# Decay attention and two MoE layers on one core: one scan chain per pair of chunks, three joins, one normalised block per chunk

## The reference, cut to what matters

```python
batch, n_heads, seq, head_dim = (4, 8, 768, 48)
mag = np.sqrt(a_re * a_re + a_im * a_im)
scale = np.minimum(mag, 0.999) / (mag + 1e-06)
a_re_n, a_im_n = (a_re * scale, a_im * scale)
for t in range(S):
    ar, ai = (a_re_n[:, :, t, :, None], a_im_n[:, :, t, :, None])
    new_re = ar * S_re - ai * S_im
    new_im = ar * S_im + ai * S_re
    S_re, S_im = (new_re + kv, new_im)      # kv: outer product of k[t] and v[t]
    y[:, :, t] = einsum('bhd,bhde->bhe', q[:, :, t], S_re)
x = y, tokens by features (3072 x 384)
h = np.maximum(np.maximum(x @ w1, x @ w2), x @ w3);  x = h @ w_out
# then a second MoE: each token to the one of 8 experts that its logits pick, times a gate
```

## Time and profile before

| | |
|---|---|
| Median of three runs | 1024.53 us |
| The profiled execution | 1025.89 us |
| Its span in the trace | 1024.0 us |
| TensorE matmul busy | 858.9 us (84% of the span) |
| VectorE busy | 649.9 us (63%) |
| GpSimd busy | 481.0 us (47%) |
| ScalarE busy | 450.2 us (44%) |
| From `y_copy(23)` to the end | 656.3 to 1024.0 us |

### The profile page before, as it was taken

The page is one execution under the profiler, slowest core; times in us unless marked ns, Lnnn a source line. Parts: engine busy times, 40 slices in busy tenths (PEclk is TensorE's granted clock), DMA queues, the critical chain, the costliest instruction groups (busy, mean ns, idle before and its releaser), DMA issues.

```text
span 1024.0 us, 18210 instructions
## 1 busy us (share of the span) xinstructions
PE 858.9 (84%) x6326; PEld 770.8 (75%) x6327; DVE 649.9 (63%) x1050; ACT 450.2 (44%) x834; POOL 481.0 (47%) x868
## 2 busy tenths in 40 slices
PE   1236576779898989979998999956999999999995
PEld 1235475678787878868897889856888888888885
DVE  5998866897797888849556665237522352546722
ACT  5751563555555545533444333222422342445621
POOL 1168988996089939963992000004221222323321
PEclk9556887889998999989999999985999999999998
DMA  9104144415233241403211111142711132415410
GB/s 297 57 19 120 51 100 112 113 65 150 77 91 92 74 98 52 102 32 85 62 37 44 37 37 38 63 176 74 278 43 34 46 121 79 157 43 171 152 38 31
DMA packets 42245, 90.78 MB, mean 89 GB/s; under 512 B 6312, under 2 KB 23728, under 8 KB 40768
## 3 DMA queue, kind: packets, MB, share of 16 engines
q1 hardware_dynamic: 38080, 77.48, 24.9%
q0 software_dynamic: 4096, 12.40, 3.8%
HBM read 70.20 MB, written 18.48 MB: 87 GB/s over the span
## 4 chain that ended last, share of the span: by engine, by line
PE 45%; POOL 23%; DVE 16%; issue 5%; DMA 5%; ACT 4%; SPq 1%; ACTq 0%; DVEq 0%; POOLq 0%
POOL c_re L1817 7%; POOL c_im L1818 6%; POOL ring L1820 5%; POOL ring L1821 5%; PE mm L1511 5%; PE yu L1511 4%; PE tr L1511 4%; PE mm L1515 4%; PE tr L1515 4%; PE tr L1512 4%; PE mm L1512 4%; PE yu L1512 4%; PE yu L1515 4%; PE mm L1736 3%; DMA ring<-an_scratch 2%
## 5 line engine op out<-in xcount | busy, mean ns | idle before, releaser
L1511 PE MATMUL mm<-up_hi,x_hi 128*128 128x384 f32 x432 | 162.0, 375 | 64.6 <-DVE h_sb L1064 45.7
L1512 PE MATMUL mm<-up_lo,x_hi 128*128 128x384 f32 x432 | 150.8, 349 | 0.0
L1511 PEld LDWEIGHTS mm<-up_hi,x_hi 128*128 128x128 f32 x432 | 84.8, 196 | 81.8 <-DVE h_sb L1064 51.5
L1817 POOL TENSOR_TENSOR c_re<-ring 112x128 f32<-112x128 f32 (+1 forms) x160 | 106.3, 665 | 67.8 <-DMA ring<-an_scratch 43.8
L1904 POOL DMA_INDIRECT out_rows<-g_o,rows_out x30 | 34.7, 1158 | 184.0 <-DVE g_o L1445 184.0
L900 ACT ACTIVATE g_h<-tr 128x512 f32<-128x512 f32 x60 | 35.9, 598 | 171.2 <-PE tr L1515 149.1
L1064 DVE TENSOR_TENSOR h_sb<-mm,h_sb 128x384 f32<-128x384 f32 x96 | 53.1, 553 | 85.3 <-PE mm L1515 83.1
L1818 POOL TENSOR_TENSOR c_im<-ring 112x128 f32<-112x128 f32 (+1 forms) x160 | 103.4, 647 | 0.0
L1515 PE MATMUL mm<-up_hi,x_lo 128*128 128x384 f32 x432 | 103.2, 349 | 0.0
L1820 POOL TENSOR_TENSOR ring<-c_re,c_im 112x64 f32<-112x64 f32 (+1 forms) x160 | 84.1, 526 | 12.5
L1512 PEld LDWEIGHTS mm<-up_lo,x_hi 128*128 128x128 f32 x432 | 85.4, 198 | 0.0
(11 more groups left out here) (223 smaller groups left out, 1998.4 us busy)
## 6 DMA issues: line engine op xcount, KB each, us to landing
raw<-in_moe_w SPq DMA_DIRECT2D x16, 1536.0 KB, 9.0
a_dn<-in_a_laid SPq DMA_DIRECT2D x20, 384.0 KB, 7.4
an_scratch<-a_dn SPq DMA_DIRECT2D x20, 384.0 KB, 2.3
ring<-an_scratch SPq DMA_DIRECT2D x20, 384.0 KB, 5.6
q_in<-in_q_laid SPq DMA_DIRECT2D x24, 224.0 KB, 3.0
k_in<-in_k_laid SPq DMA_DIRECT2D x24, 224.0 KB, 3.2
v_in<-in_v_laid SPq DMA_DIRECT2D x24, 192.0 KB, 3.3
x_scratch<-x_sb SPq DMA_DIRECT2D x24, 192.0 KB, 2.4
```

The costliest lines, as they stand in the source:

```text
L1511: nc.tensor.matmul(out, hi[:, x, :], w_hi(x), start=(x == 0), stop=False)
L1512: nc.tensor.matmul(out, hi[:, x, :], w_lo(x), start=False, stop=False)
L1817: nc.gpsimd.tensor_tensor(c_re[:, 0:count, :, :], cur, bc(prev[:, :, 0, :], 2, 2), ALU.mult).then_inc(chain_prod, 1)
```

## The change

- Every group from 2 on has its own chain of 15 steps; the double chain of two groups is gone. 157 chain steps instead of 160.
- Every group from 2 on has three joins: six more joins on VectorE (24 instructions).
- The joins of a group stand in three places. Groups 5 and up: the first behind `k_decay` in chunk 2g-3, the second behind the mask of chunk 2g-2, the third behind `k_decay` in chunk 2g-2. Groups 2 to 4: the first behind the mask of chunk 2g-2, the two others behind `k_decay` of that chunk.
- From chunk 4 on, and in chunk 2, one block is normalised in a chunk (before: two in chunks 0 to 4, then one). Block m of chunk n is n+7; the last, 23, falls in chunk 16 instead of 14.
- Ring loads of groups 4 and 6 to 11 stand one or two chunks later in SyncE's program, in chunk 2g-5.
- GpSimd: `turns(g-1)` stands behind step 12 of chain g.
- VectorE: the first late join stands ahead of `norm_inverse`; `moe_max(n-1, 1, 1)` stands ahead of the second late join and of the rotation.
- Start: blocks 2 and 3 are summed ahead of the joins of group 0 and applied (scaled) ahead of `z_newton(0)`, `q_decay(0)` and `k_decay(0)`; `up_low(0)` moves into chunk 0.

```diff
-            if g < SINGLE:
-                return ring_b[:, g % RING, :, :, :, :]
-            return ring_q[:, g // 2 % 2, :, :, :, :]
+            return ring_b[:, g % RING, :, :, :, :]
...
         def norms_in(n):
-            if n < 5:
-                return (2 * n + 4, 2 * n + 5)
-            return (n + 9,) if n + 9 < NORMS else ()
-
-        joins_early = {1: 1}
-        joins_late = {2: 2, 4: 3, 6: 4, 8: 5, 10: 6, 11: 7, 14: 8, 15: 9, 18: 10, 19: 11}
+            first = 2 * n + 4 if n < 2 else n + 6 if n < 4 else n + 7
+            count = 2 if n in (0, 1, 3) else 1
+            return tuple(m for m in range(first, first + count) if m < NORMS)
+
+        joins_early = {1: [(1, b) for b in range(7)]}
+        joins_late = {}
+        for g in range(DIRECT, NG):
+            joins_early[2 * g - 2] = [(g, 0 if g < 5 else 1)]
+            joins_late[2 * g - 2] = [(g, 1), (g, 2)] if g < 5 else [(g, 2)]
+            if g >= 5:
+                joins_late[2 * g - 3] = [(g, 0)]
...
-        ring_at = {max(g - 1, 2 * g - 7): g for g in range(DIRECT, NG)}
+        ring_at = {(g - 1 if g < 4 else 4 if g == 4 else 2 * g - 5): g for g in range(DIRECT, NG)}
...
+            norm_rsqrt(2, norm_of(2))
+            norm_rsqrt(3, norm_of(3))
             split_dn()
             act.wait_ge(s_const, 1)
             stage_z(0)
             z_square(0)
-            norm_rsqrt(2, norm_of(2))
-            z_recip(0)
-            norm_rsqrt(3, norm_of(3))
             norm_rest(2, norm_of(2))
             norm_rest(3, norm_of(3))
+            z_recip(0)
...
+                for g, number in late[:1]:
+                    join(g, number)
                 for m in norms:
                     norm_inverse(m, norm_of(m))
-                if late is not None:
-                    for number in range(apart, len(joins_of(late))):
-                        join(late, number)
+                if prev:
+                    moe_max(n - 1, 1, 1)
+                for g, number in late[1:]:
+                    join(g, number)
                 if more:
                     rotation(n + 1)
-                if prev:
-                    moe_max(n - 1, 1, 1)
...
-            for g in range(SINGLE, NG, 2):
-                if g > SINGLE:
-                    turns(g - 2)
-                chain_steps(g, range(1, 17))
-                turns(g - 1)
-                chain_steps(g, range(17, HALF // 2))
-            turns(NG - 2)
+            for g in range(DIRECT + 1, NG):
+                chain_steps(g, range(1, 13))
+                turns(g - 1)
+                chain_steps(g, range(13, BLK))
             turns(NG - 1)
```

More of the change, by code:

```diff
@@ L449, in chain_of @@
                 return ring_8[:, g, :, :, :, :]
-            if g < SINGLE:
-                return ring_b[:, g % RING, :, :, :, :]
-            return ring_q[:, g // 2 % 2, :, :, :, :]
+            return ring_b[:, g % RING, :, :, :, :]
         def steps_of(g):
             return list(chain_of(g).shape)[2] - 1
-        chains = [g for g in range(1, NG) if g < SINGLE or g % 2 == 0]
         def steps_before(g):
-            return sum(steps_of(c) for c in chains if c < g)
+            return sum(steps_of(c) for c in range(1, g))
         def joins_of(g):
@@ L467, in joins_of @@
                 return [(ring_8[:, g, b, :, :, :], ring_8[:, g, b - 1, 7, :, :]) for b in range(1, 8)]
-            if g < SINGLE:
-                return [(ring_b[:, g % RING, b, :, :, :], ring_b[:, g % RING, b - 1, BLK - 1, :, :]) for b in range(1, NBLK)]
-            return [(ring_b[:, g % RING, b, :, :, :], ring_b[:, g % RING, 1, BLK - 1, :, :]) for b in (2, 3)]
+            return [(ring_b[:, g % RING, b, :, :, :], ring_b[:, g % RING, b - 1, BLK - 1, :, :]) for b in range(1, NBLK)]
         def joins_before(g):
@@ L1181, in _ @@
                 ending = norms_in(n - 1) if 1 <= n <= NC else ()
-                late = joins_late.get(n)
-                apart = 0 if n in (2, 10) else 1
+                late = joins_late.get(n, ())
                 if prev2:
@@ L1202, in _ @@
                     norm_m2(m, norm_of(m))
-                if n in joins_early:
-                    for number in range(len(joins_of(joins_early[n]))):
-                        join(joins_early[n], number)
+                for g, number in joins_early.get(n, ()):
+                    join(g, number)
                 if n == 0:
+                    up_low(0)
                     up_low(1)
@@ L1211, in _ @@
                     up_low(2)
-                if late is not None:
-                    for number in range(apart):
-                        join(late, number)
                 if prev:
@@ L1811, in chain_steps @@
                         pool.wait_ge(pads_loaded, 16 * min(RING, max(RING - DIRECT, g - 1)))
-                        for x in range(g, g + (1 if g < SINGLE else 2)):
-                            pool.wait_ge(ring_loaded[x % RING], 32 * (x // RING + (1 if x % RING >= DIRECT else 0)))
+                        pool.wait_ge(ring_loaded[g % RING], 32 * (g // RING + (1 if g % RING >= DIRECT else 0)))
                     count = list(of.shape)[1]
```

27 lines of the change are left out of this document (8 added, 19 removed).

## The result

| | before | after |
|---|---|---|
| time, median of 4 runs (us) | 1024.4 (1023.4 to 1025.8) | 998.4 (997.2 to 999.0) |
| profiled execution: time, span (us) | 1025.9, 1024.0 | 998.1, 996.4 |
| mean granted clock of TensorE | 0.917 | 0.958 |

The ratio is 0.974 (95% interval 0.973 to 0.976): 2.6% faster, 26.0 us. The forecast was 1002, 3.6 us too high.

The account below looks back on a forecast made before the run. TensorE's floor of 21.6 us a chunk bounds the kernel, with losses above it from waits for VectorE and chains. Terms 0 - 0.6 + 12.1 + 12.0 = 23.5 us off 1025.9 gave 1002.4, forecast 1002, range 989 to 1018.

Parts of the forecast that it names:

- The start: Stretches 0 and 1: first scores about 4.5 us later, chain 1 about 5 earlier; 0 for `y_copy(1)`, bounds -3 and +4.
- stretch 2: The stretch ending at `y_copy(2)`: 32.1 us after 31.5, a loss of 0.6, with VectorE waiting for chain 2.
- Stretches 3 to 7: Chunk stretches cut at `y_copy`: 129.5 us together against 141.6 before, 12.1 gained.
- Stretches 8 to 23: Floor of 345.6 (21.6 a chunk) plus 11 us of stall: 356.6 against 368.6, 12.0 gained.
- Ten stalls for `x_lo`: In stretches 8 to 21, the late join makes `x_lo` 1.0 us late, 1.4 in odd ones; about 11 us in all.
- the surcharge: Odd stretches: VectorE enters 0.6 us late after the join behind the mask, so `x_lo` is 1.4 late instead of 1.0.
- Short idle pieces without a slow clock: Stretches 8 to 23: TensorE's short idle pieces at the late joins were priced without a slow clock.
- Free joins: Rival: first joins also fall into GpSimd's pauses, the 11 us of stall vanish: 991; chance 0.15.
- Full exclusion: Rival: a join's instructions each wait behind a chain's, 3.7 us instead of 2.65 a join: 1014; chance 0.05.
- Chains that change what they wait for: Rival: steady chains 10 us longer, groups from 6 on miss their joins: 1025, no change; chance 0.07.
- GpSimd short: Rival: chains 2, 4 and 5 miss by 3 to 5 us; stretches 2, 6 and 8 pay: 1012; chance 0.15.
- VectorE as the bound: Rival: late joins show in full and drop the clock in 12 stretches: 1043, deciding from 2.8 a stretch; chance 0.08.

Follow-up runs that it names:

- the kernel with the old table: Changed kernel with the table of blocks per chunk (two blocks in each of chunks 0 to 4) and the ring-load chunks put back: 998.9 us.
- two kernels that let joins fall into GpSimd's pauses: Changed kernel with 8 chain steps ahead of `turns`, not 12: 995.0; also each chain from 6 on waiting for the previous group's first join: 992.8.
- the last two kernels: Start undone and GpSimd held, plus group 3's joins split over three places: 986.6; then also group 4's third join behind `x_lo`: 987.6.
- one of three helpers: The start's edit; the changed kernel with the part ahead of the loop put back as before: 992.3 us.
- the main idea alone: Changed kernel with start, table of blocks and place of the maximum put back, keeping only single chains and joins in three places: 996.0 us.
- the kernels with the first join held too: Changed kernel, 8 steps ahead of `turns`, chains from 6 on waiting for the previous group's first join: 992.8; with the start undone too: 986.4.

## Why the prediction held, and where it did not

Of the 4.1 us by which the forecast of the profiled execution's span was too high (1000.5 against 996.4), 4.7 lie in stretches 8 to 23 and 0.9 in 3 to 7; the start, stretch 2 and the end give 1.5 back.

**The start** was priced at 0 for `y_copy(1)`, and that came out (+0.4). Chain 2's start at 100.3 (101.2) and stretch 2 at 32.1 (32.5) were also right, with VectorE waiting for chain 2 as forecast. Yet the edit costs 6.1 us, and the prediction calls the stretch's loss 0.6: it is the net of the late chain 2 and of the norm that the stretch loses. That without this edit the stretch would be 27.5 stands nowhere in it. A sum can be right and hide a loss of 5 beside a gain of 4.

**Stretches 3 to 7** hold one by one: 32.3, 21.4, 26.7, 21.5, 26.7 against 33.0, 22, 26.4, 21.7, 26.4, together 128.6 against 129.5. Stretch 3 is closer still than that says: its terms as written add up to 32.65, not 33.0. The reason for stretch 4, ScalarE's wait in the earlier trace rows, is borne out by the kernel with the old table, in which it came back together with 8.8 us. VectorE waited 5.4 us for chain 2; the prediction had it wait some 8 (from 129 to 137). From stretch 8 on it waited once, 0.5 us, for chain 5 at the start of stretch 8.

**Stretches 8 to 23** are the term that was mis-sized: 6.3 us over the floor instead of 11. Ten stalls for `x_lo` were forecast and ten came, but they are shorter, 5.6 us of TensorE's idle time in all. (By its own figures, 1.0 and 1.4 a stretch, the ten make 12.4, not 11.) The longest but one and the longest:

```profile
285.27 0.79 PE L1507 MATMUL mm<-up_hi,x_lo 128*128 128x384 f32 x3 [0.95 <-DVE x_lo L1048]
308.13 0.79 PE L1507 MATMUL mm<-up_hi,x_lo 128*128 128x384 f32 x3 [0.97 <-DVE x_lo L1048]
```

In stretch 9 `x_lo` ends 8.7 us behind the stretch's begin (308.08 - 299.35), where 8.8 were forecast. What was too large is the surcharge: the odd stretches were said to begin 0.6 late behind the join at the mask and to stall for 1.4. They don't. In 9 to 15 `k_t` is done 1.42 us behind the stretch's begin, in the even ones 1.28 to 1.41, and `x_lo` ends at 8.5 to 8.7 in both but for stretches 8 (9.1) and 12 (6.8, without a rotation). The odd ones from 9 to 17 lie 0.64 over the floor on average, which is about their stalls, and the even ones from 8 to 16 0.83. Of these 4.2 us only 1.8 are stalls for `x_lo`; in 10, 12, 14 and 16 TensorE also comes to its first scores later (4.34 behind the begin, against 3.83 to 4.05 in 9, 11 and 15), for a reason that no run here isolates. Stretches 8 to 17 lose 7.4 us, 19 0.7, and stretch 18 takes 19.7 us in every kernel here, before the change too, 1.9 below the floor by which it was counted. So 1.9 of the 4.7 us by which this term was off are that one stretch; the rest is the surcharge, 8.1 instead of 11. Short idle pieces without a slow clock were priced rightly (1.00 throughout).

**The rivals.** *Free joins* at 991: the mechanism is real, since two kernels that let joins fall into GpSimd's pauses gained 3.4 and 5.6 us, but in the changed kernel the first and third joins of stretches 8 to 19 ran beside a chain every time. *Full exclusion*: worked out from a step's four instructions, a join would have taken 3.7 us; with a chain beside it, it takes 2.66, without 2.00. The Trainium skill ("SBUF — State Buffer", its summary of rules for kernel authors) says that of two such instructions the second one to issue fully blocks until the first finishes. The trace again shows a part and not the sum. *Chains that change what they wait for*, and *GpSimd short*: no wait for a chain over 0.5 us from stretch 8 on; before that, the last two kernels show how little room chains 3 to 5 have, of which the prediction had said 3 us for 4 and 5. *VectorE as the bound*: even stretches stayed under 23.3 at full clock, but 1.95 us more ahead of `x_lo` was enough to bring stretches 8 to 10 to 25 to 27 and stretches 8 to 23 to 37.0 over the floor. Over the rival's 12 stretches that is 3.1 each, and by its threshold of 2.8 the change's gain is gone, as measured.

## What to carry to other kernels

Price an edit by what it costs with everything else in place and with everything else gone: here one of three helpers cost 6 us, the other two gained 10.7 us early and lost 5.5 later, where GpSimd ran beside the joins, and the main idea alone was as fast as the whole. When an edit delays something that a load waits for, follow that load to the end of the chain it feeds, even if the next milestone comes in time. Where two engines slow each other and one of them has room, let that one wait: an added wait and one changed number on GpSimd gave 5.6 us.

## What the hardware showed that was not expected

How even a join's two prices are: 2.08 us from the first start to the last end with GpSimd idle, in whichever stretch and kernel; mostly 2.7 (2.46 to 2.77) with a chain beside it all the time; and 2.34 for the third joins of stretches 9 to 17 in the kernels with the first join held too, where GpSimd is busy for 1.0 us of it. Work added on the way that bounds TensorE cost more than itself as soon as the clock fell: 1.95 us became 3.2 and 4.4 in stretches 9 and 10 (clock 0.93 and 0.87) but 1.1 in 11 and 12 (1.00), while the same kernel without it, with stalls of up to 0.97 us, kept the clock at 1.00 for sixteen stretches.
